# Token mixing run one batch ahead of its products, late reads paced, whole operands rounded at once

## What is computed

```python
def _moe2_ref(x, w_tok1, w_tok2, w_ch1, w_ch2):
    xt = x.transpose(0, 2, 1)
    h = np.maximum(xt @ w_tok1, 0.0) @ w_tok2        # over the 576 tokens, 256 wide inside
    u = x + h.transpose(0, 2, 1)
    h2 = np.maximum(u @ w_ch1, 0.0) @ w_ch2          # over the 512 channels, 1536 wide inside
    return (u + h2).astype(np.float32)
```

## Time and profile before

| | |
|---|---|
| median of 3 runs | 689.85 us (688.78 to 692.72) |
| the profiled execution's own time | 692.18 us |
| its span, first to last instruction | 690.4 us |
| mean granted clock of TensorE | 0.982 of full speed |
| busy: PE / DVE / ACT / POOL | 663.2 / 510.0 / 319.3 / 255.2 us |

### The profile page before, as it was taken

The page is one execution under the profiler, slowest core; times in us unless marked ns, Lnnn a source line. Parts: engine busy times, 40 slices in busy tenths (PEclk is TensorE's granted clock), DMA queues, the critical chain, the costliest instruction groups (busy, mean ns, idle before and its releaser), DMA issues.

```text
span 690.4 us, 17219 instructions
## 1 busy us (share of the span) xinstructions
PE 663.2 (96%) x6977; PEld 639.5 (93%) x6977; DVE 510.0 (74%) x853; ACT 319.3 (46%) x676; POOL 255.2 (37%) x318
## 2 busy tenths in 40 slices
PE   8999999999999999999969798999999899999997
PEld 7878999999999999989958698999999899999997
DVE  5469868686777768786875669887887799676763
ACT  4375562625444452626434216654546656343440
POOL 6474664846464554725478420000001111111000
PEclk9799999999999999999989899999999999999999
DMA  9861343232432332297495053567659998979784
GB/s 201 223 192 28 62 80 81 44 66 52 104 52 49 61 76 58 61 142 155 138 221 191 9 197 121 181 226 244 210 205 318 359 359 263 312 194 310 206 224 68
DMA packets 204926, 109.46 MB, mean 159 GB/s; under 512 B 163112, under 2 KB 192944, under 8 KB 204336
## 3 DMA queue, kind: packets, MB, share of 16 engines
q1 hardware_dynamic: 187888, 64.66, 37.3%
q0 software_dynamic: 7008, 38.41, 16.6%
q10 hardware_dynamic: 9952, 5.31, 3.3%
HBM read 69.41 MB, written 38.93 MB: 157 GB/s over the span
## 4 chain that ended last, share of the span: by engine, by line
PE 85%; DVE 7%; DMA 3%; issue 2%; ACT 1%; SPq 1%; POOL 0%; DVEq 0%; POOLq 0%; ACTq 0%
PE bank L967 9%; PE bank L969 8%; PE bank L968 8%; PE tq L967 3%; PE tq L968 3%; PE tq L969 3%; DMA h_rows<-hq 3%; PE bank L1586 3%; PE bank L1587 3%; PE bank L1588 3%; PE bank L843 3%; PE bank L1022 3%; PE bank L1818 3%; PE bank L1820 3%; PE bank L1819 3%; PE s L631 2%
## 5 line engine op out<-in xcount | busy, mean ns | idle before, releaser
L1778 ACT ACTIVATE ck__hi<-ck__raw 128x576 fp32r<-128x576 f32 x84 | 51.4, 675 | 64.4 <-DMA ck__raw<-h_rows 64.4
L1782 DVE TENSOR_TENSOR ck__lo<-ck__raw,ck__hi 128x576 fp32r<-128x576 f32 x84 | 59.5, 748 | 14.6 <-ACT ck__hi L1778 14.6
L1754 POOL DMA_DIRECT2D ck__raw<-h_rows x28 | 14.9, 534 | 145.5 <-PE bank L1588 49.2
L1062 POOL TENSOR_TENSOR k_lo<-kr,k_hi 128x288 fp32r<-128x288 f32 x64 | 55.2, 866 | 27.2 <-ACT k_hi L1058 27.0
L1104 DVE RECIPROCAL rg<-rg 128x288 f32<-128x288 f32 x32 | 61.5, 1923 | 0.0
L1586 PE MATMUL bank<-U__hi,W__hi 128*128 128x288 f32 x192 | 57.1, 297 | 3.9 <-ACT hq L1618 3.4
L1587 PE MATMUL bank<-U__hi,W__lo 128*128 128x288 f32 x192 | 56.6, 295 | 0.0
L1588 PE MATMUL bank<-U__lo,W__hi 128*128 128x288 f32 x192 | 56.5, 294 | 0.0
L967 PE MATMUL bank<-k_hi,WV_hi 128*128 128x288 f32 x184 | 55.5, 301 | 0.0
L968 PE MATMUL bank<-k_hi,WV_lo 128*128 128x288 f32 x184 | 54.3, 295 | 0.0
L969 PE MATMUL bank<-k_lo,WV_hi 128*128 128x288 f32 x184 | 54.1, 294 | 0.0
(11 more groups left out here) (273 smaller groups left out, 2352.4 us busy)
## 6 DMA issues: line engine op xcount, KB each, us to landing
h_rows<-hq SPq DMA_DIRECT2D x24, 1008.0 KB, 5.5
ck__raw<-h_rows POOLq DMA_DIRECT2D x28, 864.0 KB, 5.9
x_turned<-xblocks SPq DMA_DIRECT2D x16, 288.0 KB, 5.1
u_kept<-X SPq DMA_DIRECT2D x4, 1152.0 KB, 4.7
W__raw<-in_moe_w_ch POOLq DMA_DIRECT2D x6, 768.0 KB, 7.6
ub<-u_kept POOLq DMA_DIRECT2D x4, 1152.0 KB, 8.5
out_x<-ob SPq DMA_DIRECT2D x56, 72.0 KB, 5.0
vt<-in_v SPq DMA_DIRECT2D x70, 48.0 KB
```

What stands on the lines that cost most here:

```text
L1062: e.tensor_tensor(lo, t, hi.bitcast(F32), ALU.subtract).then_inc(Z.lo_done, 1)
L1782: e.tensor_tensor(lo, raw, hi.bitcast(F32), ALU.subtract).then_inc(Z.cl_done, 1)
```

## The change

- **Order of the token stage.** Products run up(0), up(1), down(0), up(2), down(1), up(3), down(2), down(3). `token_up` is cut in PE's part and the part of ACT and DVE, which stand at different places. h goes to four banks of its own (s2 for even batches, tq2 for odd), the downward products to four others; there are two h1, the second in the place of xT0; xT2 has a place of its own at U0. `first_token_down` is gone: all eight downward products wait for both h_lo. Reads `x_in(2)` and `x_in(3)` move from POOL's queue to SP's.
- **First slice of w_ch1.** It is read once the last block's upward products are done, four products earlier, and ahead of the second token weights. Its sums, ACT's seven roundings and three of DVE's subtractions move into the feed-forward part; the other four stand between the two h_lo of batch 0. The seven of the second slice are spread over the additions of down(3), the seven U_lo stand before h of batch 3.
- **Token weights.** T1 is split in pieces of 512, 512 and 256 columns instead of 1024 and 256, at `ff[-18]` to `ff[-14]` instead of -25 and -23; T2 in the token stage.
- **Late reads** wait for one step of the up stage each instead of coming together; two parts of w_ch2 come one each in the down stage, and DVE's sums of them move by one or two chunks.
- **Down stage.** An operand is split whole (1728 columns). The last operand's products are ordered by result: all three chunks of the first result, then all of the second; its additions and transposes alternate.

```diff
+    XT0 = o
...
-    xTs = [xT0, xT1, xT0, xT3]
+    xT2, _ = weights("xT2", [P, NTT * DM], U0)
+    xTs = [xT0, xT1, xT2, xT3]
...
-    h1, _ = split("h1", [P, 2 * DM], U1)
+    h1s = [split(f"h1_{i}", [P, 2 * DM], off)[0] for i, off in enumerate((U1, XT0))]
...
-    work = [s2[:, 0:512], s2[:, 512:1024], bank[6][:, :], bank[7][:, :]]
+    h_banks = [s2[:, 0:512], s2[:, 512:1024], tq2[:, 0:512], tq2[:, 512:1024]]
+    row_banks = [bank[0][:, 0:HALF], bank[1][:, 0:HALF], bank[6][:, 0:HALF], bank[7][:, 0:HALF]]
...
-    pieces2 = [parts(T1, P, 0, 4 * TOK), parts(T1, P, 4 * TOK, TOK), parts(T2, P, 0, 2 * S)]
+    pieces2 = [parts(T1, P, 0, 2 * TOK), parts(T1, P, 2 * TOK, 2 * TOK), parts(T1, P, 4 * TOK, TOK), parts(T2, P, 0, 2 * S)]
...
     def x_in(b):
...
-                e.wait_ge(Z.t1p_done, 2)
+                e.wait_ge(Z.mm_done, HP * NU)
...
-        return dict(sync=queue) if b < 2 else dict(gpsimd=queue)
+        return dict(sync=queue)
...
+    def h_bank_free(e, b):
+        if b == 0:
+            e.wait_ge(Z.x_done, ND)
+        elif b == 1:
+            e.wait_ge(Z.x2_done, DT * NU)
+        else:
+            e.wait_ge(Z.h1l_done, 2 * (b - 1))
...
     def token_up(b, m):
...
         def tensor(e):
...
-                for m_ in range(2):
-                    work_free(e, b, m_)
+                h_bank_free(e, b)
...
-                e.wait_ge(Z.tw_lo, N_T)
+                e.wait_ge(Z.tw_lo, N_T - 1)
...
-        return dict(tensor=tensor, scalar=scalar, vector=vector)
+        return dict(tensor=tensor), dict(scalar=scalar, vector=vector)
...
     def token_down(b, t, d):
...
         def tensor(e):
-            work_free(e, b, 2 + i)
-            product(e, ps, h1, cols(DM, P * d, P), T2, cols(S, HALF * t, HALF), range(2)).then_inc(Z.t2p_done, 1)
+            if i == 0:
+                e.wait_ge(Z.h1l_done, 2 * (b + 1))
+                e.wait_ge(Z.tw_lo, N_T)
+            if 8 * b + i < 4:
+                e.wait_ge(Z.x2_done, DT * NU)
+            else:
+                e.wait_ge(Z.u_done, 8 * b + i - 3)
+            product(e, ps, h1s[b % 2], cols(DM, P * d, P), T2, cols(S, HALF * t, HALF), range(2)).then_inc(Z.t2p_done, 1)
...
     def load_w1(s):
...
-                e.wait_ge(Z.mm_done, HP * NU - DT)
-                e.wait_ge(Z.lo_done, FT1 * NU)
+                e.wait_ge(Z.mm_done, HP * NU - 2 * DT)
...
     def load_w2(part):
...
             elif part == 3:
+                e.wait_ge(Z.p4_done, NQ - 3)
                 e.dma_start(tiles(W2[S3][2][:, :], NJ), w2_block(1, 0)).then_inc(Z.w2_in3, 16)
+            elif part == 4:
+                e.wait_ge(Z.p4_done, NQ - 1)
                 e.dma_start(tiles(a11_again[:, :], NJ), w2_block(0, 0)).then_inc(Z.w2_in3, 16)
-            elif part == 4:
+            elif part == 5:
...
     def load_h(n):
...
-                e.wait_ge(Z.p4_done, NJ * (B - 1))
+                e.wait_ge(Z.p4_done, NJ * (B - 1) + n)
             elif n < NCK:
-                e.wait_ge(Z.p4_done, NQ - 2)
+                e.wait_ge(Z.p4_done, NQ - 2 + 2 * (n - 2))
...
-    def chunk_parts(g):
-
-        n = g // 3
-        hi, lo, raw = [chunk(g, which) for which in range(3)]
+    def operand_parts(n):
+
+        hi, lo, raw = [t[:, :] for t in CK[n % NCK]]
...
+    def down_last():
+
+        chunks = range(21 * B - 3, 21 * B)
+
+        def tensor(e):
+            for g in chunks:
+                e.wait_ge(Z.cl_done, g // 3 + 1)
+                first = down_part(e, g, 0)
+            first.then_inc(Z.first_done, 1)
+            for g in chunks:
+                down_part(e, g, 1).then_inc(Z.chunk_done, 1)
+        return dict(tensor=tensor)
...
     def phase1():
...
-        ff[-9].append(load_w1(0))
...
-        ff[-12].append(load_second_token_weights())
+        ff[-13] += [load_w1(0), load_second_token_weights()]
...
-        for i in range(N_T):
-            ff[2 * i - 25 if i < N_T - 1 else -8].append(split_token_weights(i))
+        for i, (hi, lo) in enumerate(tw):
+            ff[i - 18].append(hi)
+            ff[i - 16].append(lo)
...
-            ff[2 * i - 14].append(x)
+            ff[2 * i - 13].append(x)
+        ff[-9] += [w1_sum(0, k) for k in range(4)]
+        ff[-4] += [w1_parts(0, i)[0] for i in range(7)]
+        ff[-2] += [w1_parts(0, i)[1] for i in range(3)]
...
     def token_stage():
...
-        steps = [w1_sum(0, k) for k in range(4)] + [x_parts(1, i) for i in range(NTT)] + his(w1[0])
-        steps += [x_blocks(3, d) for d in range(DT)] + [x_out(3)] + los(w1[0])
-        steps += [token_up(0, 0), token_up(0, 1), x_in(2), x_in(3)] + [x_parts(2, i) for i in range(NTT)] + token_rows(0)
-        steps += [keep_u(0)] + [u_sum(0, k) for k in range(4)]
-        steps += [token_up(1, 0), token_up(1, 1), load_w1(1)] + his(u0) + [x_parts(3, i) for i in range(NTT)]
-        steps += token_rows(1) + los(u0)[:3] + [keep_u(1)]
-        steps += [token_up(2, 0), token_up(2, 1)] + [w1_sum(1, k) for k in range(4)]
-        steps += los(u0)[3:] + token_rows(2) + [keep_u(2)] + his(w1[1])
-        steps += [token_up(3, 0), token_up(3, 1), load_w1(2)] + los(w1[1])[:3] + token_rows(3) + los(w1[1])[3:]
+        steps = products(0) + products(1) + [x_in(2)] + [x_blocks(3, d) for d in range(DT)] + [x_out(3), x_in(3)]
+        steps += [x_parts(1, i) for i in range(NTT)] + [tw_hi, tw_lo, h(0, 0)] + los(w1[0])[3:] + [h(0, 1)]
+        steps += [x_parts(2, i) for i in range(NTT)] + [h(1, 0), h(1, 1)]
+        steps += rows[0] + [keep_u(0)] + products(2) + [x_parts(3, i) for i in range(NTT)] + [h(2, 0), h(2, 1)]
+        steps += rows[1] + [keep_u(1), load_w1(1)] + products(3) + [u_sum(0, k) for k in range(4)]
+        steps += his(u0) + los(u0) + [h(3, 0), h(3, 1)]
+        steps += rows[2] + [load_w1(2), keep_u(2)] + [w1_sum(1, k) for k in range(4)] + his(w1[1])
+        for i, step in enumerate(rows[3]):
+            steps += [step] + los(w1[1])[i:i + 1]
...
-        extra[22] += [load_h(2)] + [chunk_parts(g) for g in range(3)]
-        extra[23] += [load_h(3)] + [chunk_parts(g) for g in range(3, 6)]
-        extra[24] += [load_u(0), load_w2(4), w2_parts(A12)]
+        extra[22] += [load_h(2)] + [operand_parts(0)]
+        extra[23] += [load_w2(4)] + [operand_parts(1)]
+        extra[24] += [load_u(0), load_h(3), w2_parts(A12)]
...
     def down_stage():
...
-            if g == 3:
-                steps.append(load_w2(5))
+            if g in (3, 6):
+                steps.append(load_w2({3: 5, 6: 6}[g]))
...
-            if g in (1, 6):
-                steps.append(w2_sum({1: S3, 6: S4}[g]))
-            elif g in (3, 9, 13):
-                steps.append(w2_parts({3: S3, 9: S4, 13: A22}[g]))
-            while made < min(chunks, g + LEAD + 1):
-                steps.append(chunk_parts(made))
+            if g in (2, 8):
+                steps.append(w2_sum({2: S3, 8: S4}[g]))
+            elif g in (4, 10, 14):
+                steps.append(w2_parts({4: S3, 10: S4, 14: A22}[g]))
+            while made < min(7 * B, (g + LEAD) // 3 + 1):
+                steps.append(operand_parts(made))
```

More of the change, by code:

```diff
@@ L1391, in tensor @@
                             c0 = TOK * (NTT - 1) + P * m_
-                            e.matmul(work_bank(b, m_), T1[w][r, c0:c0 + P], xT[x][r, t0:t0 + DM], start=i == 0, stop=False)
+                            e.matmul(h_bank(b, m_), T1[w][r, c0:c0 + P], xT[x][r, t0:t0 + DM], start=i == 0, stop=False)
                 product(e, ps, T1, cols(TOK, P * m, P), xT, cols(DM, 0, DM), range(NTT - 1), start=False,
@@ L1419, in vector @@
                 e.tensor_tensor(x, ps, x, ALU.add).then_inc(Z.u_done, 1)
[L1420 to L1435 removed]
+            return dict(tensor=tensor, vector=vector)
         def token_rows(b):
[L1438 removed]
+            return [token_down(b, t, d) for t in range(2) for d in range(DT)]
         def keep_u(b):
@@ L1798, in down_free, with down_part @@
             e.wait_ge(Z.added, 14 * b_ + 2 * i_ + d + 1)
+        def down_part(e, g, d):
+            b, i, k = g // 21, g // 3 % 7, g % 3
+            onto = i not in (0, 1, 3)
+            xh, xl = chunk(g, 0), chunk(g, 1)
+            wh, wl = W2[i][:2]
+            ps = down_bank(b, i, d)
+            if k == 0:
+                down_free(e, b, i, d)
+            for m in range(2):
+                w = slice(2 * P * (2 * k + m) + P * d, 2 * P * (2 * k + m) + P * (d + 1))
+                x = slice(HALF * m, HALF * (m + 1))
+                e.matmul(ps, wh[:, w], xh[:, x], start=not onto and k == 0 and m == 0, stop=False, skip_group_check=onto)
+                e.matmul(ps, wl[:, w], xh[:, x], start=False, stop=False, skip_group_check=onto)
+                last = e.matmul(ps, wh[:, w], xl[:, x], start=False, stop=k == 2 and m == 1, skip_group_check=onto)
+            return last
@@ L1800, in down_chunk @@
         def down_chunk(g):
             b, i, k = g // 21, g // 3 % 7, g % 3
-            xh, xl = chunk(g, 0), chunk(g, 1)
-            wh, wl = W2[i][:2]
             def tensor(e):
```

(35 more changed lines are left out.)

77 lines of the change are left out of this document (33 added, 44 removed).

## The result

The changed kernel takes 668.25 us (median; 666.16 to 672.84, four executions) beside 691.29 us of the kernel before on the same chip (688.78 to 695.12, four): ratio 0.967, 95% interval 0.960 to 0.975. Two later comparisons gave medians of 671.0 against 688.71 (ratio of the means 0.972, 0.967 to 0.976) and 666.91 against 689.96 (0.968, 0.963 to 0.974). One execution of the first of the two, 676.13, counts as slow and stands outside its ratio. All 16 executions of the changed kernel lie between 665.45 and 676.13, with a median of 669.1. The prediction was 667.5.

A forecast was written before the change was run, and what follows sets the result against it. PE was taken as the bound, busy 663.2 of 690.4 us, so only its stops and half clock could be regained. Terms summed to 23.1 us, giving 666.8 at the median's level; plus 0.7 made 667.5 us, range 663.5 to 675.

The forecast's parts named there:

- The last feed-forward block: Before the token stage: T1 in 512-column pieces, placed later, ends PE's waits for xk_lo; gain 1.4 us (0 to 1.4).
- Token stage: From T, the first token product, to the up stage: PE runs through in 53.1 us; gain 15.7 us (10 to 16.4).
- The 0.7 us that I added: Token stage: allowance for a short wait at rows(0) or rows(3), the downward products of batches 0 and 3.
- The first rival: Token stage, rows(0): DVE waits out POOL's operations, PE stands 3.3 us; 670 to 673 us, chance 0.13.
- The second rival: Token stage: first slice's read comes no sooner, up(1) starts 2 us late, rows(0) 3 more; 673 to 675 us, chance 0.12.
- Start of the up stage and late reads: Up stage: W_lo spread over rows(3) gains 2.3 us; reads paced to one a step, shortening hq writes, gain 3.4 us.
- The sign that I gave: Up stage: hq writes under 8 us would show the forecast right.
- Whole operands: Down stage: 28 roundings and subtractions each instead of 28 x 3, ready 3.6 us after the read lands; cost 0.
- the third rival: Down stage, from the fifth operand: reads landing later than 11.4 us after issue starve PE; up to 696 us, chance 0.02.
- the sentence on what is late next: Late reads: DVE's sums of a_again and S4 move one or two chunks, still seven and ten chunks ahead of use.
- Tail: End of the kernel: only the first wait after SP's twelve stores goes; gain 0.3 us (0 to 1).

The follow-up runs named there:

- the early slice: Changed kernel with the read of W1's second slice issued ahead of the two u_kept writes of rows 0 and 1: 676.08 us.
- the version with all three edits: Changed kernel plus earlier last h_rows read, earlier read of W1's second slice and eight small prologue products: 671.13 us against 666.91 of the changed kernel.

## Why the prediction was right, by its steps

- *The last feed-forward block*: -1.4 taken, -1.9 measured. The waits went as described. They cost more than their idle time: at the two stops the starts of matmuls lie 1.38 and 0.57 us apart, where 0.13 is usual, so 1.7 us in all. Undoing the pieces of T1 alone brought the whole 1.9 back.
- *Token stage*: -15.7 taken, -17.0 measured, outside the upper bound of 16.4. The whole stage is pure work, and that is 51.89 and not 53.1: I had counted 6.66 for a set of eight downward products, where 48 matmuls at the usual 0.133 need 6.4. The 0.7 us that I added for a short wait at rows(0) or rows(3) didn't come either. Each input came as worked out: the slice's sums at T - 5.4 (T - 6 taken), xT1 at T - 1.0 (T - 1), the second h_lo at T + 12.5, the upper value of 8.5 to 12.5. The seven U_lo ran with POOL idle, as taken. This term and the clock of the prologue (-3.6) are why the profiled execution, at 666.2, came out under the 669.1 worked out for one like it.
- *The first rival* (DVE slower beside POOL) did not come at rows(0), though the second h_lo came only 0.6 us before it was needed. My price of 1.26 us for a W_lo was a mean over those that met a subtraction of POOL and those that didn't, and the rival's 1.6 us for one of POOL's already held its waits for DVE. One by one, the four W_lo took 1.17, 0.68, 1.78 and 1.78 us. Where the two engines meet, a W_lo and one of POOL's subtractions follow each other every 1.70 us, and alone they come every 0.60 and 1.25 us, 1.85 together. With the early slice, a U_lo and a sum come every 1.77 us, alone every 0.67 and 1.25, 1.92 together. So in both places it is one after the other, but for 0.15 us a pair. The Trainium skill ("SBUF — State Buffer", section "SBUF: two separate sides") has the shared port pair as an exclusive lock for a whole instruction; within that 0.15 us the trace agrees. What it doesn't give is the rival's time, since not every subtraction of DVE met one of POOL's.
- *The second rival* (the slice's read comes no sooner) did not come, and undoing the early read shows that its price was right: 673 to 675 us taken, 673.89 measured in one execution.
- *Start of the up stage and late reads*: -5.7 taken, -5.4 measured. Undoing the pacing alone costs 5.6 us, not 3.4: the stops it brings back (3.8 us) also cost the clock. The 2.3 us stop is gone, and of the 3.4 us a stop of 0.2 is left, behind the write of 8.9 us. The sign that I gave, writes under 8 us, didn't hold: they take 7.2 to 8.9, and in other executions of the same kernel up to 10.8, with a stop of 1.8 us.
- *Whole operands*: 0 taken. The durations were right (1.65 for 1.67, 1.95 for 1.97, landing 5.9), and no read of an operand took over 10.1 us, so the third rival's 11.4 was not reached. But the cost on DVE's order was left out: see the next point. Undoing them alone costs 1.7 us, most of it the half clock behind a longer stop.
- **The step that failed** is the sentence on what is late next: that a_again and S4 move "by one or two chunks with them, seven and ten chunks ahead of use", and cost nothing. Ahead of use they are. But DVE does them in the same queue as the additions that free PE's banks, and it had 0.1 us of idle time in that stretch before. In the changed kernel it stood 2.9 us there, 1.7 of them for reads and 0.6 for ACT's rounding of a moved sum, and PE stood 1.7 us and lost 2.2. I had looked at the deadline of the sums and not at what else stands behind and in front of them on their engine. Which of the moves costs how much is not shown: with every late read of the up stage at its old time DVE still stood 2.6 us.
- *Tail*: -0.3 taken, -0.4 measured.

The sum of the parts was right within 0.7 us because -1.8 on two terms met +2.2 on the one that failed. That is luck, and so in part is the median's 0.75 us: the three medians of this kernel are 666.9, 668.25 and 671.0.

## What to carry to other kernels

Put the next batch's independent products in front of the ones that wait, and make sure that the first of them has its inputs: here 11.2 us went when the order was undone, and 7.3 when the early read was. When a read is made later, don't stop at the deadline of its data; ask what stands behind the work on it in its engine's queue, and whether that engine has idle time there. Work on DVE and on POOL that reads SBUF should be kept from meeting, even if it means a later read.

## What the runs showed that I had not expected

- TensorE's granted clock in the first 40 us of the same code was 1.00, 0.96 or 0.87 by execution. With a little more work in one gap of the prologue the mean of the execution was 0.996 or more in six of six; in the version with all three edits, which has the same work there, it was 0.993 to 1.00, with stops later on.
- After stops of 2.15, 2.4, 2.5, 2.7, 2.9 and 4.2 us PE ran for some us at 1.2 GHz; after stops of 1.8, 1.9 and 2.1 us, and after the 2.3 us of the earlier trace rows, it did not. After 1.95 us it did in the version with all three edits, and did not in the kernel before: the length of a stop alone doesn't decide.
- U_lo cost 1.8 us beside POOL's sums and 0.7 alone, while DVE's additions out of the banks kept their 0.46 us beside POOL.
- The write of 1 MB took 4.2 us just ahead of the late reads and 5.1 to 11.3 us beside them, as long as its slot was used again. At the same step of the same code it took 5.1, 7.1 and 8.3 us in three executions. In a kernel whose slack there is zero, that is its spread.
